# Hybrid attention and two MoE layers: the first batch's decays on two engines, sign planes moved, fillers moved

## What is computed

```python
mag = np.sqrt(a_re * a_re + a_im * a_im)
scale = np.minimum(mag, 0.999) / (mag + 1e-06)
a_re_n, a_im_n = (a_re * scale, a_im * scale)
for t in range(S):                       # S = 768, batch 4, heads 8, head_dim 48
    new_re = ar * S_re - ai * S_im       # ar, ai: a_re_n, a_im_n of token t
    new_im = ar * S_im + ai * S_re
    S_re, S_im = (new_re + k_t v_t^T, new_im)
    y[:, :, t] = q_t @ S_re
x = soft_moe(y)                          # 8 experts of 4 slots, softmax over tokens and over slots
out = square(relu(x @ w_in)) @ w_out     # 3072 tokens, 384 -> 2048 -> 384
```

## Time and profile before

| | before |
|---|---|
| median of 3 runs | 688.62 (686.57 to 689.92) |
| profiled execution, its own time | 689.71 |
| span of its trace | 687.8 |
| mean granted TensorE clock | 0.952 |
| busy: TensorE matmul, VectorE, ScalarE, GpSimd | 517.2, 412.6, 328.7, 146.5 |
| first instruction of the product chain | 38.6 |
| first matmul on attention data | 112.4 |
| attention, experts, MLP end at about | 424, 464, 688 |

### The profile page before, as it was taken

How to read it: one execution, slowest core, us unless ns; L and a number is a source line. 1 busy time by engine, 2 the same in 40 slices (tenths; PEclk the granted TensorE clock), 3 DMA queues, 4 the chain that set the end, 5 groups by cost and what they waited for, 6 DMA issues and landing times.

```text
span 687.8 us, 11763 instructions
## 1 busy us (share of the span) xinstructions
PE 517.2 (75%) x4548; PEld 394.9 (57%) x4548; DVE 412.6 (60%) x673; ACT 328.7 (48%) x568; POOL 146.5 (21%) x128
## 2 busy tenths in 40 slices
PE   1000008797587975959876998999999999999997
PEld 1000004575465754747665785447888888888885
DVE  1399995999699996978944321438633333332321
ACT  3877052464455644312323233147755556565653
POOL 5001000100001000010000000006655655555553
PEclk9999999899688997879989999999999999999999
DMA  6040065372563625375799889940010101010001
GB/s 244 0 138 0 2 179 108 81 162 51 137 195 81 162 46 117 83 206 155 189 219 262 192 273 426 438 194 1 2 46 1 47 0 47 1 46 1 18 29 46
DMA packets 39558, 79.59 MB, mean 116 GB/s; under 512 B 7120, under 2 KB 28752, under 8 KB 37200
## 3 DMA queue, kind: packets, MB, share of 16 engines
q1 hardware_dynamic: 36192, 62.33, 32.3%
q10 hardware_dynamic: 3312, 16.52, 7.4%
HBM read 55.12 MB, written 4.72 MB: 87 GB/s over the span
## 4 chain that ended last, share of the span: by engine, by line
PE 53%; DVE 19%; DMA 8%; ACT 7%; SPq 6%; issue 4%; POOL 2%; ACTq 0%; DVEq 0%; POOLq 0%
PE ps L1214 10%; PE ps L1215 9%; PE ps L1216 9%; DMA stk<-xout 8%; PE ps L959 7%; SPq L253 4%; PE ps L1196 3%; PE ps L945 2%; DVE tt L668 2%; DVE big L673 2%; DVE tt L670 2%; DVE xout L764 2%; SPq L263 2%; PE ps L1116 2%; PE ps L1138 2%
## 5 line engine op out<-in xcount | busy, mean ns | idle before, releaser
L615 POOL TENSOR_TENSOR hlo<-qs,hhi 128x512 fp32r<-128x512 f32 x96 | 127.1, 1324 | 125.0 <-DVE qs L929 121.7
L929 DVE TENSOR_TENSOR qs<-rs 128x512 f32<-128x512 f32 x96 | 75.1, 783 | 129.1 <-ACT rs L552 129.0
L945 PE MATMUL ps<-ident 128*32 128x512 bf16 x256 | 74.0, 394 | 90.9 <-DMA stk<-xout 90.9
L959 PE MATMUL ps<-stk 112*128 112x224 f32 (+1 forms) x384 | 91.4, 403 | 55.1 <-DMA stk<-xout 39.0
L959 PEld LDWEIGHTS ps<-stk 112*128 112x128 f32 x384 | 81.1, 233 | 67.0 <-DMA stk<-xout 44.1
L1214 PE MATMUL ps<-hhi,who 128*128 128x512 f32 x288 | 112.1, 389 | 1.6 <-POOL hlo L615 1.6
L1215 PE MATMUL ps<-hlo,who 128*128 128x512 f32 x288 | 112.0, 389 | 0.0
L1216 PE MATMUL ps<-hhi,wlo 128*128 128x512 f32 x288 | 112.0, 389 | 0.0
L552 ACT ACTIVATE rs<-ps 128x512 f32<-128x512 f32 x96 | 57.4, 598 | 84.0 <-PE ps L1196 83.8
L945 PEld LDWEIGHTS ps<-ident 128*32 128x32 bf16 x256 | 20.5, 97 | 112.6 <-DMA stk<-xout 91.2
L602 POOL MEMSET big<- 128x2304 f32 x4 | 8.2, 2039 | 285.0 <-DVE big L673 285.0
(11 more groups left out here) (149 smaller groups left out, 809.2 us busy)
## 6 DMA issues: line engine op xcount, KB each, us to landing
stk<-xout SPq DMA_DIRECT2D x144, 128.0 KB, 3.8
wt<-in_w SPq DMA_DIRECT2D x10, 1536.0 KB, 12.2
xq<-in_xq SPq DMA_DIRECT2D x24, 384.0 KB, 5.2
wt<-in_w ACTq DMA_DIRECT2D x6, 1536.0 KB, 8.6
big<-in_a_all ACTq DMA_DIRECT2D x9, 768.0 KB, 7.2
vr<-in_v_all SPq DMA_DIRECT2D x24, 192.0 KB, 4.2
out<-ost SPq DMA_DIRECT2D x6, 768.0 KB, 3.5
wins<-in_w_in SPq DMA_DIRECT2D x1, 3072.0 KB, 17.2
```

What stands on the lines that cost most here:

```text
L615: pool.tensor_tensor(hlo[:, i % NHS, :], qs[:, i % NQS, :], hhi[:, i % NHS, :].bitcast(F32), ALU.subtract).then_inc(lo_ready, 1)
L929: dve.tensor_tensor(qs[:, i % NQS, :], rs[:, i % NQS, :], rs[:, i % NQS, :], ALU.mult).then_inc(sq_ready, 1)
L945: nc.tensor.matmul(ps[P - SL:P, bank, :], idb[:, 0:SL], idle, start=True, stop=True)
L959: last = nc.tensor.matmul(ps[:, h // 2, h % 2 * SK:h % 2 * SK + cols], x[:, 0:CH], x[:, CH:CH + cols], start=True, stop=True)
```

## The change

Four things are done. (1) For batch 0, ScalarE waits for two constants only and squares the real planes of thirds 0 and 1; VectorE waits for none, squares the other four planes (`first_squares`), adds them, and makes the overshoots (`first_overshoot`). Small Square and Sqrt instructions on one column stand where they make ScalarE load these tables. `excess` and `normalise` of batch 0 alternate by third. The wait for all constants follows the decays. (2) `signs(b)`, which holds the sign planes and the raw loads of the next batch, moves from the head of pass b to the last chunk of pass b - 1, ahead of `copy_y`, `copy_x` and `copy_raw` there; for batch 0 it stands ahead of the loop. (3) On VectorE the cuts of the product chain in pass 1 are shifted by `shift`, so that more of it comes in the early chunks. (4) Ten fillers instead of fourteen wait for the first key product instead of `stack(0)`, and the six ahead of `scores(0)` are gone.

```diff
--- before.py
+++ after.py
@@ -180,7 +180,7 @@
         ld_raw = [sem(f"ld_raw{t}") for t in range(DT)]
         ld_xq = [sem(f"ld_xq{k}") for k in range(NXQ)]
         ld_v = [sem(f"ld_v{k}") for k in range(NV)]
-        squares, m2_ready, mag_ready, over_ready = sem("squares"), sem("m2_ready"), sem("mag_ready"), sem("over_ready")
+        squares, own_squares, m2_ready, mag_ready, over_ready = sem("squares"), sem("own_squares"), sem("m2_ready"), sem("mag_ready"), sem("over_ready")
         log_ready, inv_ready, p_ready, an_ready = sem("log_ready"), sem("inv_ready"), sem("p_ready"), sem("an_ready")
         sm_ready, m_ready, signed = sem("sm_ready"), sem("m_ready"), sem("signed")
         chain, weighed, kq_ready, rot_ready = sem("chain"), sem("weighed"), sem("kq_ready"), sem("rot_ready")
@@ -314,7 +314,7 @@
 
         @block.scalar
         def _(act):
-            act.wait_ge(consts, NCONST)
+            act.wait_ge(consts, 2)
 
             def load_raw(b, t):
                 act.wait_ge(an_ready, DT * (b - 1) + t + 1)
@@ -327,10 +327,13 @@
 
             def take_squares(b, t):
                 act.wait_ge(ld_raw[t], 16 * (b + 1))
-                if b:
-                    act.wait_ge(an_ready, DT * (b - 1) + t + 1)
-                    act.wait_ge(sm_ready, DT * (b - 1) + t + 1)
-                    act.wait_ge(m_ready, 2 * b)
+                if b == 0:
+
+                    nc.scalar.activation(grid(U_ + t * PT, [1, PT]), grid(RAW + t * PT, [1, PT]), ACT.Square).then_inc(squares, 1)
+                    return
+                act.wait_ge(an_ready, DT * (b - 1) + t + 1)
+                act.wait_ge(sm_ready, DT * (b - 1) + t + 1)
+                act.wait_ge(m_ready, 2 * b)
                 nc.scalar.activation(grid(U_ + t * PT, [1, PT]), grid(RAW + t * PT, [1, PT]), ACT.Square).then_inc(squares, 1)
                 nc.scalar.activation(grid(V_ + t * PT, [1, PT]), grid(RAW + PF + t * PT, [1, PT]),
                                      ACT.Square).then_inc(squares, 1)
@@ -445,23 +448,29 @@
                     act.wait_ge(stored[t % 2], 16 * (t // 2))
                 nc.scalar.activation(ost[:, t % 2, k, :], ps[:, 2 + 3 * (t % 2) + k, :], ACT.Copy).then_inc(acc_copied, 1)
 
-            for t in range(DT):
+            def signs(b):
+                for t in range(DT):
+                    sign_planes(b, t)
+                    if b < B - 1:
+                        load_raw(b + 1, t)
+
+
+            nc.scalar.activation(rescale[:, 0:1], eps[:, 0:1], ACT.Square)
+            for t in range(DT - 1):
                 take_squares(0, t)
+            nc.scalar.activation(rescale[:, 1:2], eps[:, 0:1], ACT.Sqrt)
             for t in range(DT):
                 magnitude(0, t)
             for t in range(DT):
                 log_mag(0, t)
-                overshoot(0, t)
             for t in range(DT):
                 inv_mag(0, t)
+            act.wait_ge(consts, NCONST)
+            signs(0)
             for p in range(B + 1):
                 for c in range(NC + 3 * (p == B)):
                     n = (p - 1) * NC + c
                     if c == 0 and p < B:
-                        for t in range(DT):
-                            sign_planes(p, t)
-                            if p < B - 1:
-                                load_raw(p + 1, t)
                         norm_squares(p)
                     if p == B - 1 and 2 <= c < 5:
                         if c == 2:
@@ -495,6 +504,8 @@
                         copy_flipped(2 * pair)
                     if 0 <= n < NT and has_turn(n):
                         copy_kt(n, 1)
+                    if c == NC - 1 and p < B - 1:
+                        signs(p + 1)
                     if 1 <= n <= NT:
                         copy_y(n - 1)
                     if pair is not None:
@@ -621,9 +632,25 @@
                 return off + j // 2 * 2 * NC + j % 2
 
             def norm2(b, t):
-                dve.wait_ge(squares, 2 * (DT * b + t + 1))
+                if b == 0:
+                    dve.wait_ge(squares, min(t + 1, DT - 1))
+                    dve.wait_ge(own_squares, t + 1 + (t == DT - 1))
+                else:
+                    dve.wait_ge(squares, DT - 1 + 2 * (DT * (b - 1) + t + 1))
                 u = grid(U_ + t * PT, [1, PT])
                 dve.tensor_tensor(u, u, grid(V_ + t * PT, [1, PT]), ALU.add).then_inc(m2_ready, 1)
+
+            def first_squares(t):
+
+                dve.wait_ge(ld_raw[t], 16)
+                for c in range(t < DT - 1, 2):
+                    x = grid(RAW + c * PF + t * PT, [1, PT])
+                    dve.tensor_tensor(grid((V_ if c else U_) + t * PT, [1, PT]), x, x, ALU.mult).then_inc(own_squares, 1)
+
+            def first_overshoot(t):
+                dve.wait_ge(mag_ready, t + 1)
+                dve.tensor_scalar(grid(R_ + t * PT, [1, PT]), grid(U_ + t * PT, [1, PT]), -0.999, 0.0, ALU.add,
+                                  ALU.max).then_inc(over_ready, 1)
 
             def excess(b, t):
                 dve.wait_ge(inv_ready, DT * b + t + 1)
@@ -814,22 +841,28 @@
                     if total * lo < ends[k] <= total * hi:
                         part(b, k)
 
-            dve.wait_ge(consts, NCONST)
+            def shift(p, x):
+
+                return x + (p == 1 and 0 < x < 1) * 0.06 * (1 - x)
+
             for t in range(DT):
+                first_squares(t)
                 norm2(0, t)
             for t in range(DT):
+                first_overshoot(t)
+            for t in range(DT):
                 excess(0, t)
-            for t in range(DT):
                 normalise(0, t)
             for t in range(DT):
                 scaled_mag(0, t)
+            dve.wait_ge(consts, NCONST)
             for p in range(B + 1):
                 if 1 <= p < B:
                     for t in range(DT):
                         normalise(p, t)
                 for c in range(NC + 1 * (p == B)):
                     n = (p - 1) * NC + c
-                    lo, mid, hi = c / NC, (c + 0.5) / NC, (c + 1) / NC
+                    lo, mid, hi = [shift(p, (c + x) / NC) for x in (0, 0.5, 1)]
                     if 0 <= n < NT:
                         weigh(n)
                         key_query(n, 0)
@@ -1057,13 +1090,14 @@
                 nc.tensor.matmul(y_ps[:, u, :], xsb[:, 0, 0:P], ident[:], start=True, stop=True)
             for k in range(KM):
                 nc.tensor.matmul(ps[:, 4, k * P:(k + 1) * P], xsb[:, 0, 0:P], ident[:], start=True, stop=True)
-            pe.wait_ge(stacked[0], 96)
-            keep_busy(14)
+            pe.wait_ge(kq_ready, 1)
+            keep_busy(10)
             for n in range(NT + 3):
                 full = n < NT - NC
                 pair = n // 2 - 2 if n >= 4 and n % 2 == 0 else None
                 if n < NT:
-                    keep_busy(6 if full else 1)
+                    if n:
+                        keep_busy(6 if full else 1)
                     scores(n)
                 if pair is not None:
                     flip(2 * pair)
```

## The result

The changed kernel takes 667.7 (667.4 to 671.8, four runs) against 689.3 (686.6 to 692.6, four runs) for the kernel before on the same chip; the ratio is 0.9699, 95% interval 0.9642 to 0.9756. The profiled execution took 667.75 with a span of 666.0, 21.8 less than before's 687.8. From here on "after" is the changed kernel.

The account below looks back on a forecast made before the run. Attention was taken as bound by a relay of VectorE, restack transfer and TensorE, the MLP by TensorE. Terms -8.65 - 4.05 + 0.25 - 11.7 = -24.2 gave 665.5 profiled, 664.5 median, stated as 665; 8-in-10 range 660 to 676.

Parts of the forecast that it names:

- Stretch A: Decays of batch 0: product chain starts at 30.0 instead of 38.6; -8.65, bounds -7 to -9.5.
- Stretch B: Pass 1: scores(0) starts 6.4 earlier without fillers ahead but runs slower; -4.05, bounds -3 to -6.
- the argument on chunk 4: Pass 1: the shifted cuts fill 1.35 of VectorE's wait, lost again in chunk 4, where mask(3) comes late.
- Stretch C: Pass 2: the 5.92 wait for sign planes goes but is all given back, stack(6) landing behind raw loads; +0.25.
- the bound of -3.2: Pass 2's best case: stack(6) lands as without raw loads, last issue at 184 and 3.9 for the piece.
- The rival in which queues take turns: Pass 2: raw loads and restack served in turn, restack in at about 189; -2, total 26.5, time 662; chance 0.08.
- Stretch D: Pass 3 on: waits of 5.46 for sign planes and 4.23 and 2.03 in chunk 14 go; -11.7, bounds -5 and -13.
- the weight load's catch of stack(14): Chunk 14: the load, 0.75 behind the last issue, would be 2.7 behind, removing VectorE's waits of 4.23 and 2.03.
- stacks 15 and 16 would meet the loads as before: Behind stack(14): these restacks meet the weight loads as now and land 12 or more earlier.
- the fourth rival: Passes 3 and 4: weight loads catch restacks they now miss, about 7.5 each; +6, time 695; chance 0.02.
- Rival 3: Sign planes gain nothing anywhere, leaving the decays and pass 1: 12 to 13, time 676; chance 0.15.
- Rival 1: Chunk 14: stack(14) is still caught by the weight load; -5.5 there, total 18, time 671; chance 0.22.

Follow-up runs that it names:

- e3_fillers: Kernel before with the fillers alone moved (ten from the first key product on, none ahead of scores(0)), no shifted cuts; 683.2, ratio 0.9898.
- e5_no_shift: Changed kernel with the old cuts of the product chain in pass 1; 667.6, ratio 0.9710.
- e6_back2: Changed kernel with the sign planes and raw loads of batch 2 put back to the head of pass 2; 666.1, ratio 0.9685.
- e9: Changed kernel with raw loads of batches 2 and 3 issued only when the pass's first restack has landed; 658.0, ratio 0.9566.
- e12: Changed kernel with the raw loads of batch 3 alone (pass 2) waiting for the restack's landing; 666.3, ratio 0.9688.
- e2_signs: Kernel before with the sign planes and the raw loads in their loop moved alone; 681.6, ratio 0.9896.
- e10: Kernel of e9 with the first three weight loads one chunk earlier on ScalarE; 662.2, ratio 0.9604.
- e1: Kernel before with the decays of batch 0 alone changed; 678.7, ratio 0.9838.
- e8: Kernel before with the first weight load alone moved behind the landing of stack(14); 687.6, ratio 0.9993.
- e11: Kernel before with raw loads of batches 2 and 3 alone moved behind the landing of the pass's first restack; 682.8, ratio 0.9897.
- e7: Changed kernel with the sign planes of batch 3 alone put back to the head of pass 3; 672.2, ratio 0.9779.
- The three parts alone: Kernel before with one part each: decays of batch 0 (678.7), sign planes with raw loads (681.6), fillers without shifted cuts (683.2).
- e4: Changed kernel with raw loads of batches 2 and 3 put behind norm_squares in ScalarE's program; 669.1, ratio 0.9715.

## Why the prediction was nearly right

**Stretch A, -8.65 forecast, -8.0 measured.** The path ran as written, through the last sum, root, logarithms and exponentials. The term that was too short is the start: the raw transfers of thirds 1 and 2 landed at about 8.0 and 10.1 instead of 7.5 and 9.7, and VectorE, which began third 1 at 8.12, was free for the last squares at 10.1 too, so that the last sum ended at 13.1 instead of 12.5. The tables that were loaded ahead decided nothing: the root's was in place at 10.3, and the last root waited till 13.12 for VectorE.

**Stretch B, -4.05 forecast, -4.0 measured.** scores(0) started at the landing after 8.77 without work, and took 5.22. The fillers kept nothing awake; what paid is that twenty no longer stood behind the landing. e3_fillers gives about the same 4 without the shift (4.2 at stack(2), 3.5 at stack(6)), and e5_no_shift, with 81.0 from stack(0) to stack(6) against 82.0, shows no gain from the shift, as the argument on chunk 4 said.

**Stretch C, +0.25 forecast, +0.2 measured.** This is the reading that a look at VectorE's waits alone misses: 5.9 was taken away and nothing came of it. stack(6) behind three raw loads, after:

```profile
L253 SPq DMA_DIRECT2D stk<-xout x6: 551/602/697, 168.4 to 172.0; - x6
...
DMA to landing us min/median/max: 6.5/6.8/7.5
```

Every piece took 6.5 to 7.5, where the earlier trace rows has 3.3 in the median, and the restack was in 11.2 after its first issue (forecast 11.6). The wait then turned up at the masks (0.60 and 1.30) and at the sums of batch 3 (2.59, 0.51, 0.51), the two places named: 5.5 of the 5.9. e6_back2 undoes it without loss; e9 and e12 let the restack go first and the 3.4 appears, near the bound of -3.2. The rival in which queues take turns, with the landing near 8.7 after the first issue and C at -2, has lost. What each queue moved shows why. These are the DMA queues (packets, MB, share of 16 engines) in the 3.6 from the first issue of stack(6) to its last, first after (168.4 to 172), where no other queue moved anything, then before, where no raw loads were ahead (180.35 to 183.95); q10 is ScalarE's queue and q1 SyncE's:

```profile
q10 hardware_dynamic: 296, 0.86, 76.4%
```

```profile
q1 hardware_dynamic: 445, 0.41, 41.9%
```

So the raw loads moved 0.86 MB and the restack nothing, where it moved 0.41 MB before. Its first data came between 172.6 and 173, and the raw loads were nearly through at 174. e2_signs and e5_no_shift show the same (0.90 and 0.93 MB of raw loads, nothing of the restack, in the like stretch); why theirs then lands after 12.3 and not 11.2 stays open. The rule of the Trainium skill's "DMA: Bandwidth & Descriptors" (arbitration) is about rows for which an engine has work. The trace does not show whether the restack's work had reached the DMA engines while only raw data moved, so these runs decide against the landing near 8.7 and not about that rule.

**Stretch D, -11.7 forecast; -12.0 up to stack(16), then +2.0 given back.** The number of the first part was right and part of its mechanism was not. As forecast, the first weight load went out 2.9 behind stack(14)'s last issue (forecast 2.7), no piece took over 3.9, and scores(14) started at the landing. The stretch from 12 to 16 takes 42.0 in every kernel in which batch 3's sign planes were moved (e10, with its loads moved, 44.0), and otherwise 42.0 and VectorE's waits: before 5.46 + 4.23 + 2.03 = 11.7, e1 5.58 + 2.33 = 7.9, e3 5.12 + 2.62 = 7.7, e8 5.42 + 2.48 = 7.9, e11 4.94 + 2.75 + 1.14 = 8.8, e7 5.19 + 0.48 = 5.7, against 12.0, 8.2, 7.9, 8.0, 9.1 and 5.9 in the table. The sign planes' wait, 4.9 to 5.6, is the part that always goes.

The step that failed is that the 4.23 and 2.03 in chunk 14 were put down wholly to the weight load's catch of stack(14). With the load far away (e8) VectorE still waited 2.48 there, so that the catch accounts for 3.8 of the 6.26, and the median did not move. Nor does the distance alone make a catch. In five traces the load follows the last issue by 0.7 to 0.9, and the slowest piece took 9.0 (before), 7.5 (e11), 4.8 (e1), 4.6 (e3) and 3.9 (e7). The kernel before was traced once, so how often it is caught isn't known. That the sum came out at 11.7 is luck in so far as it rests on this one trace: held against a stretch of 50, as in e1, e3 and e8, the same change is worth 8. The medians of e1 and e3, 2.4 and 2.0 better than expected, hint that other executions of before have some of it too; e8's median hints against it.

What stands in chunk 14 without a catch is TensorE, early at its scores, idle 3.0 to 3.3 for the restack, and then slow through them (6.1 to 6.3). After, VectorE and with it the restack are 5.5 earlier there, beyond what the stretches ahead gave, and TensorE only 3.3 (read at scores(12)), so that TensorE arrives with the restack (0.16) and takes 3.29. The 2.3 to 2.6 of e1, e3 and e8 are what besides the sign planes can be gained without a catch; that TensorE's later arrival is the cause is argued from these rows, no run set it by itself.

The second step that failed is that stacks 15 and 16 would meet the loads as before. stack(16) was issued 2.1 behind its load, instead of 1.0, and was in 13.8 after its first issue instead of 11.6; scores(16) took 4.91 instead of 3.29. In pass 4 scores(19) took 4.98 instead of 3.29. This is the fourth rival in small, 1.8 instead of 30, but that the loads cost it is not shown: in e5_no_shift and e6_back2 the load is just as far ahead (2.0 and 2.1), stack(16) was in after 12.3 and 11.6, scores(16) took 3.29, and from stack(16) to scores(23) they have 88.0 and 89.7 against 88.7 before and 90.5 after.

**The total.** -24.2 forecast against -21.8 in the profiles and -21.6 in the medians; 665 against 667.7, in the range of 660 to 676. 0.7 of the miss is A's start, 2.0 what came back behind stack(16). Rival 3, no gain from the sign planes, is out by e7_back3. Rival 1, with 5.5 for D, is out for the changed kernel, where stack(14) is not caught. The three parts alone gave -10.4, -7.5 and -6.0 in the medians, 24 together, which within their intervals (3 to 4 each way) is what all of them gave.

## What to carry to other kernels

A wait that is taken from an engine is worth what the next latest input leaves of it; look at which transfers the moved instructions carry along, and what is issued right behind them. Where a small restack is on the path, let bulk loads wait for its landing: one wait, put on a queue that has nothing to do until then, was worth 9.7 here, about as much as the largest part of the change by itself (10.4 for the decays), and 5.5 in the kernel before (e11), where VectorE's wait for the sign planes stood behind it. And a wait in one profiled execution can be that execution's: before a term of the sum rests on a collision, look into more than one execution, and ask what wait would be left without it.

## What the runs showed of the hardware

A transfer instruction on ScalarE's queue did not wait for the activations ahead of it in the program (e4: raw loads issued at 85.37 and from 85.95, activations running from 85.79 to 90.1).

A restack issued 1.2 behind the last of three raw loads moved nothing in its first 3.6, while the loads moved 0.86 MB; without loads ahead it had moved 0.41 MB by then (after against before, stack(6)).

The granted clock at the start of the experts was full in twelve of the fourteen traces and lower in two, after much the same work; why is open. These are windows of TensorE, columns: stretch, length, then busy time of TensorE, its weight loads, VectorE, ScalarE, GpSimd, granted clock, DMA share, GB/s; first e9_raws_landed, then after.

```profile
380.00:392.00 12.00, 9.30 (x117) 5.89 (x113) 0.42 (x1) 5.93 (x18) 0.74 (x1) 1.00 1.00 424
392.00:400.00 8.00, 8.00 (x44) 4.77 (x48) 5.01 (x9) 0.84 (x1) 0.29 (x1) 0.57 1.00 421
```

```profile
391.00:403.00 12.00, 9.31 (x118) 5.86 (x112) 0.42 (x1) 5.94 (x18) 0.74 (x1) 1.00 1.01 424
403.00:411.00 8.00, 7.98 (x66) 4.49 (x66) 5.01 (x9) 1.44 (x2) 0.29 (x1) 1.00 1.01 429
```

In the 12 ahead TensorE had been busy 9.30 and 9.31; then it was granted 0.57 (between 1.2 and 2.4 GHz) in the one and 1.00 (2.4 GHz) in the other, and did 44 matmuls in 8 instead of 66. In e9_raws_landed and e6_back2, the two with the low clock, the table's "rest" is 282 instead of 279: 3.2 that comes with the clock and not with an edit.
